# A block inverse by one 64-column product per doubling step, in a reordered schedule

## The reference

```python
for t in range(S):
    kt, vt, bt = (k_n[:, :, t], v[:, :, t], beta[:, :, t, None])
    y[:, :, t] = np.einsum('bhd,bhde->bhe', q[:, :, t], state)
    v_old = np.einsum('bhde,bhd->bhe', state, kt)
    state = state + bt[:, :, :, None] * np.einsum('bhd,bhe->bhde', kt, vt - v_old)
...
for e in range(E):
    h = np.maximum(x @ w1[e], 0.0)
    out += p[:, e:e + 1] * (h @ w2[e])
...
gate = 1.0 / (1.0 + np.exp(-(x @ w_gate)))
return (gate * (x @ w_val) @ w_out).astype(np.float32)
```

## Time and profile before

| | us |
|---|---|
| median of 3 runs | 1728.94 (1724.21 to 1731.8) |
| the profiled execution, its own time | 1731.9 |
| span of its trace | 1730.1 |
| start to first slot | 23.66 |
| slot 0 | 32.38 |
| slot 1 | 39.71 |
| slot 4, a steady one | 41.69 |
| slot 11, the last | 39.23 |
| end of the last slot to the end | 1219.6 |

### The profile page before, as it was taken

The page is one execution under the profiler, slowest core; times in us unless marked ns, Lnnn a source line. Parts: engine busy times, 40 slices in busy tenths (PEclk is TensorE's granted clock), DMA queues, the critical chain, the costliest instruction groups (busy, mean ns, idle before and its releaser), DMA issues. The chain is left out here.

```text
span 1730.1 us, 41911 instructions
## 1 busy us (share of the span) xinstructions
PE 1686.0 (97%) x18182; PEld 1504.5 (87%) x18182; DVE 627.4 (36%) x1169; ACT 442.5 (26%) x852; POOL 205.7 (12%) x309
## 2 busy tenths in 40 slices
PE   6999999999997999999999999999989999999999
PEld 4888888888896899899999999999978888888887
DVE  4766666666642232222222222222243222222221
ACT  3343333343321211211122111111143222222222
POOL 2532222222220300200003000000000000000000
PEclk9999999999998999999999999999999999999999
DMA  6435444434225633111221111121021000000000
GB/s 131 75 83 120 100 90 88 98 87 98 58 58 161 222 109 120 63 37 36 102 81 37 66 44 64 37 73 37 0 82 56 19 1 19 19 0 18 0 19 19
DMA packets 171757, 113.68 MB, mean 66 GB/s; under 512 B 82224, under 2 KB 151216, under 8 KB 171600
## 3 DMA queue, kind: packets, MB, share of 16 engines
q1 hardware_dynamic: 171600, 111.33, 22.8%
HBM read 92.44 MB, written 18.87 MB: 64 GB/s over the span
## 5 line engine op out<-in xcount | busy, mean ns | idle before, releaser
L1184 DVE SCALAR_TENSOR_TENSOR hl<-ebank,hh 128x512 fp32r<-128x512 f32 x168 | 116.4, 693 | 500.8 <-ACT hh L1149 500.8
L1149 ACT ACTIVATE hh<-ebank 128x512 fp32r<-128x512 f32 x168 | 100.6, 599 | 576.4 <-PE ebank L1215 576.4
L1213 PE MATMUL ebank<-w2l,hh 128*128 128x384 f32 x672 | 226.3, 337 | 2.3 <-DVE hl L1184 2.3
L1215 PE MATMUL ebank<-w2h,hh 128*128 128x384 f32 x672 | 226.3, 337 | 0.0
L1214 PE MATMUL ebank<-w2h,hl 128*128 128x384 f32 x672 | 225.5, 336 | 0.0
L1213 PEld LDWEIGHTS ebank<-w2l,hh 128*128 128x128 f32 x672 | 126.2, 188 | 9.9 <-DVE hl L1184 3.0
L1214 PEld LDWEIGHTS ebank<-w2h,hl 128*128 128x128 f32 x672 | 126.2, 188 | 5.9
L1215 PEld LDWEIGHTS ebank<-w2h,hh 128*128 128x128 f32 x672 | 126.0, 188 | 0.0
L1409 DVE TENSOR_TENSOR prod<-gbank,gate 128x512 f32<-128x512 f32 x72 | 49.8, 691 | 209.3 <-ACT gate L1356 209.3
L1213 PE MATMUL ebank<-room,w1h 128*128 128x512 f32 x252 | 99.2, 394 | 4.3 <-DVE w1l L1171 4.3
L1215 PE MATMUL ebank<-room,w1h 128*128 128x512 f32 x252 | 100.5, 399 | 0.0
(11 more groups left out here) (180 smaller groups left out, 3344.0 us busy)
## 6 DMA issues: line engine op xcount, KB each, us to landing
room<-x_hi SPq DMA_DIRECT2D x12, 768.0 KB, 4.3
room<-x_lo SPq DMA_DIRECT2D x12, 768.0 KB, 5.8
xh<-x_hi SPq DMA_DIRECT2D x12, 768.0 KB, 4.3
xl<-x_lo SPq DMA_DIRECT2D x12, 768.0 KB, 5.8
brep<-in_beta SPq DMA_DIRECT2D x24, 256.0 KB, 6.0
k_raw<-in_k SPq DMA_DIRECT2D x12, 384.0 KB, 4.7
v_raw<-in_v SPq DMA_DIRECT2D x12, 384.0 KB, 6.1
q<-in_q SPq DMA_DIRECT2D x12, 384.0 KB, 7.0
```

Source lines behind the costliest of these rows:

```text
L1149: nc.scalar.activation(hs[i][0][:, :], bank[i][:, :], ACT.Relu).then_inc(hh_done, 1)
L1184: nc.vector.scalar_tensor_tensor(out=hs[i][1][:, :], in0=bank[i][:, :], scalar=0.0, in1=hs[i][0][:, :].bitcast(F32), op0=ALU.max, op1=ALU. ...
L1213: mm(dst, stat[0], mov[1], start=first, stop=False)
L1215: return mm(dst, stat[0], mov[0], start=False, stop=last)
```

## The change

The doubling is made a recurrence on two matrices at once. X' is the inverse so far (transposed) and Y' its product with I + A; the two lie side by side in one buffer XY, 64 columns for each head. Each step masks Y' (with the identity's diagonal in the mask), transposes the masked Y' to Yn, and one product of Yn with the pair gives both the next X' and the next Y'. There are five groups for each half instead of nine (`l0` to `l4`), the unit-matrix products are gone, every product is a group of its own (start and stop both set), and I is added to A before it is rounded to Ah. Around it:
- The first X' is no longer made by TensorE: a step `first` in `pre` has GpSimd mask Ah (four 32x256 products for each half, L538) and VectorE transpose the result. It is run at the end of the slot before.
- In each of `l0` to `l3` VectorE masks from PSUM and transposes, and ScalarE, which waits for the mask, copies PSUM to XY: 256 columns in `l0` and `l3`, 512 in `l1` and `l2`. In `l4` ScalarE copies and VectorE transposes once.
- Ah is made by VectorE with a 128x1024 SCALAR_TENSOR_TENSOR (256 A + 256 I); ScalarE's copy is gone.
- The slot's order is written anew. GpSimd's splitting of the expert weights (`split`) moves from slot 0 to slot 1, behind `unit`.

```diff
+            tiles("l0", 0)
+            r("u0", 0)
+            tiles("l0", 1)
+            moe("weigh", m - 1, 0)
             n("square")
             down(m - 1, 1, 0, 1)
+            tiles("l1", 0)
             r("u0", 1)
+            tiles("l1", 1)
             down(m - 1, 1, 2, 3)
+            tiles("l2", 0)
+            moe("weigh", m - 1, 1)
+            r("au_a", 0)
+            tiles("l2", 1)
             n("norm")
             n("unit", 0)
             n("unit", 1)
+            up(0)
             moe("low", m, 0)
+            tiles("l3", 0)
+            r("au_b", 0)
+            tiles("l3", 1)
             up(1)
             moe("low", m, 1)
+            tiles("l4", 0)
             r("au_a", 1)
+            tiles("l4", 1)
...
+            tiles("m64z", 0)
+            down(m, 0, 0, 1)
+            tiles("m64z", 1)
             r("y", 1)
             pre("product_q", w, p, 0)
             r("s", 0)
             pre("product_q", w, p, 1)
+            down(m, 0, 2, 3)
             r("s", 1)
+            n("first", 0)
+            n("first", 1)
             n("turn_q", 0)
             n("turn_q", 1)
...
+                    if step == "first":
+                        pool.wait_ge(ah_done, 2 * w + which + 1)
...
+                        for b in range(NB):
+                            mask = level_mask[quarter(b), 0:BLK].unsqueeze(1).to_broadcast([BLK, HH, BLK])
+                            last = nc.gpsimd.tensor_tensor(XY[which][quarter(b), :, 0, :],
+                                                           Ah[p][quarter(b), half(which), quarter(b)], mask, ALU.mult)
+                        last.then_inc(x1_done, 1)
...
+                        act.wait_ge(lv_rdy, 10 * w + 2 * n + hf + 1)
+                        if n < 4:
+                            act.wait_ge(yt_done, 8 * w + 2 * n + hf + 1)
+                        if n == 0:
+                            copy(XY[hf][:, :, 1, :], compact_y(hf)).then_inc(xy_done, 1)
+                        elif n < 3:
+                            copy(XY[hf][:, :, :, :], pair_xy(hf)).then_inc(xy_done, 1)
...
+                        nc.vector.tensor_tensor(Yt[hf][:, :, :], y, mask, ALU.mult).then_inc(yt_done, 1)
+                        dve.wait_ge(yt_done, 8 * w + 2 * n + hf + 1)
+                        nc.vector.transpose(Yn[hf][:, :, :], Yt[hf][:, :, :]).then_inc(yn_done, 1)
...
+                        nc.vector.scalar_tensor_tensor(out=Ah[p][:, half(which), :], in0=A32[p][:, half(which), :],
+                                                       scalar=ASC, in1=eye.unsqueeze(1).to_broadcast([P, HH, P]),
+                                                       op0=ALU.mult, op1=ALU.add).then_inc(ah_done, 1)
...
+                                if n == 0:
+                                    dst, moving = yb[rows, h, :], Ah[p][rows, HH * hf + h, rows]
+                                elif n < 4:
+                                    dst, moving = pair_xy(hf)[rows, h, :, :], XY[hf][rows, h, :, :]
+                                else:
+                                    dst, moving = xb[rows, h, :], XY[hf][rows, h, 0, :]
+                                last = mm(dst, Yn[hf][rows, h, :], moving, start=True, stop=True)
```

More of the change, by code:

```diff
@@ L22 @@
 ASC = 256.0
[L23 removed]
+LEVELS = (1, 2, 4, 8, 16)
 NL = len(LEVELS)
@@ L42, in constant_tables @@
         "mask": after,
-        "pair_mask": small_eye - below(1) / ASC,
     }
     f16 = {
-        "eye": eye,
+        "eye": ASC * eye,
         "small_eye": np.tile(small_eye, (1, HH)),
-        "level_mask": np.concatenate([-below(s) / ASC for s in LEVELS], 1),
+        "level_mask": np.concatenate([(small_eye - above(s)) / ASC for s in LEVELS], 1),
     }
@@ L110, in delta_rule_attention @@
         Ah = [sb(f"Ah{i}", [P, WH, P], F16) for i in range(2)]
[L111 to L114, removed]
+        XY = [sb(f"XY{i}", [P, HH, 2, BLK], F16) for i in range(2)]
+        Xn = [sb(f"Xn{i}", [P, HH, BLK], F16) for i in range(2)]
+        Yt = [sb(f"Yt{i}", [P, HH, BLK], F16) for i in range(2)]
+        Yn = [sb(f"Yn{i}", [P, HH, BLK], F16) for i in range(2)]
+        Xa = XTb = sb("Xab", [P, WH, DP], F16)
         Y64 = sb("Y64", [P, WH, DP], F16)
@@ L303, in run @@
                                 ("turn", 0), ("turn", 1), ("product", 0), ("product", 1),
-                                ("turn_q", 0), ("turn_q", 1)):
+                                ("first", 0), ("first", 1), ("turn_q", 0), ("turn_q", 1)):
                 pre(step, 0, 0, which)
@@ L542, in pre @@
                                                 ALU.mult).then_inc(ku_done, 1)
+                        if w == 2 and which == 1:
+                            split()
+                            pool.wait_ge(w_split, 4)
                 def rec(step, w, p, o):
@@ L616, in pre @@
                         copy(KQ[p][:, four(which), 1, :], wide(bank[which])).then_inc(tq_done, 1)
-                    if step == "product":
-                        act.wait_ge(ap_done, 4 * w + 2 * which + 2)
-                        past(act, my_rdy, 4 * (w - 1))
-                        copy(Ah[p][:, half(which), :], A32[p][:, half(which), :], ASC).then_inc(ah_done, 1)
                 def moe(step, m, f, part=1):
@@ L724, in pre @@
                                                 brep[p][:, four(which), :], ALU.mult).then_inc(kb_done, 1)
+                    if step == "first":
+                        dve.wait_ge(x1_done, 2 * w + which + 1)
+                        nc.vector.transpose(Yn[which][:, :, :], XY[which][:, :, 0, :]).then_inc(yn_done, 1)
                     if step == "product":
```

193 lines of the change are left out of this document (67 added, 126 removed).

## The result

| | before | changed |
|---|---|---|
| median of 20 runs each, us | 1733.69 (1724.21 to 1745.67) | 1720.01 (1706.87 to 1730.9) |
| ratio, 95% interval | | 0.9917 [0.9892, 0.9943] |
| profiled execution, span, mean clock | 1731.9, 1730.1, 0.992 | 1725.09, 1723.3, 0.983 |

The changed kernel is 0.8% faster: 13.7 us, not 29.4, and its median lies outside my range (4.8 us of the distance from 1699.5 to 1720.0 come from a before that measured higher here than in the three runs shown, 1733.7 for 1728.9). Ratios compare executions within 1.5% of a kernel's fastest, which leaves out a single one, the profiled one of experiment 9.

What follows compares the result with a forecast made beforehand. TensorE's own list was taken to bound each attention slot. Slots 2 to 10 give 21.6, slot 1 1.0, start-up and slot 0 1.5, slot 11 5.4: 29.5 us, median 1728.94 to 1699.4, say 1699.5; range 1683 to 1715.

Steps and rivals of the forecast that it cites:

- The wide groups: TensorE's six 64-column level groups in each slot: 0.35 us each, 2.1 us added.
- the narrow ones: TensorE's `l0` and `l4` groups, `y` groups by shape: 4 x 0.30 = 1.2 us added in each slot.
- The wait at `product_q`: TensorE waits for VectorE's QK masks before the second half: 1.05 us each slot, 1.5 in slot 11.
- VectorE's queue: Level rounds, first half of a slot: VectorE's 10.8 us end before TensorE needs them at 11.5, 0.7 to spare.
- the third rival: VectorE's queue becomes the bound of the slot's first half: gain 18 us, time 1711; chance 0.15.
- The steady slot: Slots 2 to 10: 3.5 us saved less 1.05 + 0.1 of waits, say 2.4, becoming 39.3 us.
- slot 11's own fall: The 6.9 us at 1.2 GHz in slot 11 was expected to be gone.
- small waits: TensorE's small waits, such as `first`'s transpose standing behind the last state addition: 0.1 us a slot.
- Start-up and slot 0: Half 1's first group starts at 26.05, slot 0 has five level rounds instead of nine: ends 1.5 us earlier.
- the clock term: Slot 11: `up` enters the stretch of short groups, so the clock's fall goes, 6.9 / 2 = 3.4 us gained.
- The fourth rival: `product_q` wait and missing unit-matrix columns thin TensorE's work, clock falls once each slot: 1735 us; chance 0.08.
- A second step: The x for a slot's `up` is stored after the previous slot's `ylo` half 1, over 10 us ahead.

Runs made afterwards that it cites:

- experiment 9: Changed kernel with SyncE's load of the second expert's weights issued one slot later, at slot 4 instead of slot 3; 1716.73 us, ratio 0.9871.
- experiment 3: Changed kernel with four 256-column unit-matrix products, whose result nothing reads, put back ahead of each of the ten level groups; 1728.39 us, ratio 0.9949.
- experiment 4: Changed kernel with eight 256-column products of constants run during the wait ahead of `product_q`'s second half; 1722.1 us, ratio 0.9924.
- experiment 1: Changed kernel with `down(m, 0, 2, 3)` put between the halves of `product_q`; 1733.37 us, ratio 0.9976.
- 8: Changed kernel with `y` half 1 and `product_q` half 0 earlier, `s` half 1 ahead of `down`, and `au` steps before `up` behind slot 11; 1687.45 us.
- experiment 2: Changed kernel with `y` half 1 ahead of `m64z` half 0 and `product_q` half 0 ahead of `down`; 1701.27 us, ratio 0.9796.
- 5: Kernel of experiment 2 with the last slot's `au` steps ahead of the first `up` behind slot 11; 1699.22 us, ratio 0.9777 against before.
- experiment 7: Changed kernel with four 256-column unit-matrix products put back ahead of the two `l0` groups only; 1724.98 us, ratio 0.9938.
- 10: Changed kernel with `y` half 1 and `product_q` half 0 earlier and `s` half 1 ahead of `down`, old order behind slot 11; 1694.53 us, ratio 0.9752.
- 6: Changed kernel with `s` half 1 ahead of `down(m, 0, 2, 3)` at the end of the slot; 1712.22 us, ratio 0.9847.

## Why the prediction was wrong

**Right, by its steps.** The wide groups cost 0.34 to 0.35 (0.35 taken) and the narrow ones 0.30. (The Trainium skill, page "TensorE: Matmul & The Clock Gate", section "Back-to-back issue gap", would have both at the same 60 cycles; the trace doesn't bear that out.) VectorE's operation of 1024 columns took 1.23 and 1.38 in slot 5 and 1.30 in the median (1.2), GpSimd's masks 0.66 (at most 0.7). The wait at `product_q` was 0.92 (1.05) in slots 1 to 10 and 1.53 in slot 11 (1.5). VectorE's queue held; the third rival is out (by its own numbers its gain would have been 29.5 - 10.5 = 19, not 18). The steady slot is 39.2 to 39.4 (39.3), and slot 11's own fall is gone: 33.02, 5.55 less than before, against 5.4.

**Small misses.** Charging 0.1 for small waits was too little: 0.36 at `l0` in every slot and up to 0.24 at `u0` in about half of them, made up by 3.8 instead of 3.5 off TensorE's work. Start-up and slot 0 lost 0.4 us where I gave them 1.5. The first group of half 1 came at 26.81 and not at 26.05, the clock rose 3.9 us later than before (31.2 for 27.3) and fell again at 38.0 for 3.4.

**The step that failed** is the clock term: "The new order brings `up` into that stretch, so I expect the fall to be gone: 6.9 / 2 = 3.4." The fall went, but I took it for a matter of that one stretch and let the clock stand everywhere else. Over all executions the changed kernel loses 12.8 us more to it. In place of +3.4 the term measures about -10, and this explains some 14 of the 15.7 us by which the gain fell short. The trace of before was a usual one in what it lost (14.4 us, the median being 14.7), but it had one execution's falls, and I took their places for fixed. The fourth rival, at 0.08, had the right kind of mechanism. Of its two conditions the missing unit-matrix columns are borne out (experiment 3) and the wait at `product_q` is not (experiment 4); and its fall in each slot came in two of the first ten, at some 4.7 us each with the idleness beside it.

**A second step**, in the same profile: "The x that `up` of a slot needs is stored after `ylo` half 1 of the slot before, over 10 us ahead." That is so for slots 1 to 11, where TensorE never waited for x. Behind slot 11 it isn't. The last store of x is issued at 489.45 and `up` could have begun at 495.87; x came 1.60 later, and the clock fell for 17.1 us right behind. The falls at 526.1 and 543.2, of 6.8 each, are there before too. 1.6 of waiting and 17.1 / 2 = 8.5 of clock make 10.1, of the 9.4 that this part lost; a later wait there was 0.5 shorter (3.59 at 527.52 for 4.06). I had no term for it at all.

**What brings the clock down.** Shown: the loss to the clock follows the list of TensorE. One `down` moved by 2 us raises it by some 20 us (experiment 1, 27.5 to 48.6), the old unit-matrix columns cut it by a third (3), and with the three moves it is below that of before (8). Also shown: the wait at `product_q`, which I suspected first, isn't its cause (4).

In the profiled executions of the changed kernel and its ten variants the clock fell 23 times between the start of slot 1's `u0` and the end of slot 11. I find them in two places only. Fifteen begin 0.9 to 2.3 us into a slot (experiments 1, 2, 3, 5, 7 and 9). Eight stand at an idle time inside a group: each of the seven of 1.1 us or more has a fall that begins within 2.2 us of its end, and the eighth is that of 0.55 in experiment 1.

*Idle times inside a group.* Their source can be named further than "issue". All twelve traces together have 14 idle times above 0.25 us in slots 1 to 11 that stand inside a group and have no releaser. Every one of them ends 2.2 to 2.6 us after a 16 KB packet of the kind "instruction" starts (2.31 and 2.46 in the changed kernel), and in slot 3 they grow with the time at which it comes: none above 0.25 us with the packet 4.1 us into the slot (experiment 9), 0.26 with 6.0 (8), 1.45 with 7.2 (5), 1.90 with 7.6 (changed and 10). (Experiment 1 has 7.7 and no idle time, but its clock was at half there, so it worked through its list more slowly.) So TensorE most likely stood without instructions until a late packet had come. What made it late is argued: in slot 3 the load of the second weights stands for it (9), in slot 10 nothing here does. Not shown either is that the idle time makes the clock fall, though it did so seven times of seven.

*The stretch across the boundary.* Only argued: that its thinness is the cause of the fifteen. There are none in the three kernels that have `s` ahead of `down` (6, 8, 10), but none in the changed kernel's and experiment 4's own traces either, and experiment 7 speaks against it. Open: why the same rows are followed by a fall in one slot and not in the next.

## What to carry to other kernels

Making TensorE's list shorter by taking out cheap wide products can take away work that kept its clock up, as it did here. Before such a change is costed, collect the mean clock of many executions of before and price a few more falls at half their length; one trace shows one draw. Then use the work that is left to cover the new waits: here moving two groups ahead of independent work (experiment 2) took 18.7 us off the changed kernel's median, more than the 13.7 of the whole rewrite.

## What the runs showed of the hardware

- Executions of one program on one core differ by up to 1.4%, and nearly all of it is TensorE's clock: 20 executions of the changed kernel had mean clocks from 0.976 to 0.994 and times from 1730.9 to 1706.9, 1.4 us from a straight line.
- The clock can fall to half and stay there for 27.3 us while TensorE is busy for all 27.30 of them (experiment 9), with no idle time above 0.36 us in the 7 us ahead (and one of 0.92 just before that).
- TensorE can stand still for 1.1 to 2.0 us in the middle of a group that waits for no semaphore. This happened between 139 and 146 us in five of these kernels, in four of them at the same product, and in slot 10 of two. Each time TensorE went on 2.2 to 2.6 us after a 16 KB packet of the kind "instruction" had started, and each time the clock fell near it. In the kernel that has the same list and loads the second weights later it was gone from slot 3 and there again in slot 10, so that load can't be the only reason.
